# Output products of one weight block: high-part passes first, low-part passes last

## The reference, cut to what matters

```python
x = irfft(soft_threshold(rfft(x) @ (w_r, w_i) + b))   # 2 x 3008 x 256
h = x @ w_in;  g = max(h, 0) + alpha * min(h, 0);  x = g @ w_out         # layer 1, 256 -> 2048 -> 256
h = x @ w_in;  g = h if h >= 1, 0 if h <= -1, else (h + 1)**2 / 4; out = g @ w_out   # layer 2
```

## Time and profile before

| What | Value |
|---|---|
| Median of 3 runs | 1186.69 us (1186.18 to 1186.71) |
| The profiled execution: its own time | 1185.84 us |
| Its span | 1184.0 us |
| PE busy | 1172.3 us, 99% of the span |
| DVE, ACT, POOL busy | 885.6, 852.2, 693.0 us |
| Passes on TensorE | 6948 |

### The profile page before, as it was taken

The page is one execution under the profiler, slowest core; times in us unless marked ns, Lnnn a source line. Parts: engine busy times, 40 slices in busy tenths (PEclk is TensorE's granted clock), DMA queues, the critical chain, the costliest instruction groups (busy, mean ns, idle before and its releaser), DMA issues.

```text
span 1184.0 us, 21005 instructions
## 1 busy us (share of the span) xinstructions
PE 1172.3 (99%) x6948; PEld 1134.6 (96%) x6948; DVE 885.6 (75%) x1680; ACT 852.2 (72%) x1879; POOL 693.0 (59%) x724
## 2 busy tenths in 40 slices
PE   8999999999999999999999999999999999999998
PEld 2799999999999999999999999999999999999998
DVE  4687777777777777777778777777777787878775
ACT  2335567777777777777767788888878787878776
POOL 3006647667575766666556566665657575756553
PEclk9999999999999999999999999999999999999999
DMA  8687620211111201202005500000000000000000
GB/s 298 232 272 243 195 63 18 77 41 54 41 58 63 68 28 41 93 29 68 19 1 179 191 23 2 27 1 27 1 28 1 27 1 27 1 27 1 14 14 27
DMA packets 41580, 77.61 MB, mean 66 GB/s; under 512 B 4608, under 2 KB 21120, under 8 KB 41472
## 3 DMA queue, kind: packets, MB, share of 16 engines
q1 hardware_dynamic: 39392, 69.78, 17.6%
q10 hardware_dynamic: 2080, 6.48, 1.6%
HBM read 45.97 MB, written 30.28 MB: 64 GB/s over the span
## 4 chain that ended last, share of the span: by engine, by line
PE 93%; POOL 3%; DMA 1%; SPq 1%; issue 1%; ACT 1%; DVE 0%; POOLq 0%; ACTq 0%
PE bank L1170 81%; PE bank L1137 6%; PE bank L1156 2%; PE bank L1147 2%; PE bank L1122 2%; POOL g_lo L519 2%; DMA x_sb<-x 1%; POOL x_sb L465 1%; PE bank L1111 1%; POOL prep_raw L545 0%; SPq L328 0%; POOL xc_lo L495 0%; ACT prep_hi L798 0%; ACT g_hi L775 0%; SPq L334 0%
## 5 line engine op out<-in xcount | busy, mean ns | idle before, releaser
L519 POOL TENSOR_TENSOR g_lo<-g_sb,g_hi 128x376 fp32r<-128x376 f32 x510 | 506.3, 1004 | 365.8 <-ACT g_hi L775 365.2
L1170 PE MATMUL bank<-g_hi,w_out_hi 128*128 128x376 f32 x1024 | 344.9, 337 | 0.9 <-POOL g_lo L519 0.4
L1170 PE MATMUL bank<-g_lo,w_out_hi 128*128 128x376 f32 x1024 | 341.9, 334 | 0.0
L1170 PE MATMUL bank<-g_hi,w_out_lo 128*128 128x376 f32 x1024 | 341.7, 334 | 0.0
L1170 PE MATMUL bank<-xc_hi,w_in_hi 128*128 128x376 f32 x896 | 302.0, 337 | 0.0
L1170 PE MATMUL bank<-xc_hi,w_in_lo 128*128 128x376 f32 x896 | 300.3, 335 | 0.0
L1170 PE MATMUL bank<-xc_lo,w_in_hi 128*128 128x376 f32 x896 | 298.5, 333 | 0.0
L775 ACT ACTIVATE g_hi<-g_sb 128x376 fp32r<-128x376 f32 x512 | 261.1, 510 | 42.7 <-DVE g_sb L976 27.3
L1170 PEld LDWEIGHTS bank<-g_hi,w_out_hi 128*128 128x128 f32 x1024 | 192.4, 188 | 9.1 <-POOL g_lo L519 7.4
L1170 PEld LDWEIGHTS bank<-g_hi,w_out_lo 128*128 128x128 f32 x1024 | 192.4, 188 | 0.0
L1170 PEld LDWEIGHTS bank<-g_lo,w_out_hi 128*128 128x128 f32 x1024 | 192.3, 188 | 0.0
(11 more groups left out here) (83 smaller groups left out, 1534.5 us busy)
## 6 DMA issues: line engine op xcount, KB each, us to landing
gc<-group_consts SPq DMA_DIRECT2D x24, 256.0 KB, 4.4
zt<-slots_scratch SPq DMA_DIRECT2D x24, 256.0 KB, 3.8
inverse_scratch<-v_sb SPq DMA_DIRECT2D x24, 256.0 KB, 2.9
ut<-inverse_scratch SPq DMA_DIRECT2D x16, 384.0 KB, 5.1
slots_scratch<-a_sb ACTq DMA_DIRECT2D x15, 384.0 KB, 4.6
out<-y_tile SPq DMA_DIRECT2D x30, 188.0 KB, 1.9
prep_raw<-wpack SPq DMA_DIRECT2D x16, 256.0 KB, 2.6
x_sb<-x SPq DMA_DIRECT2D x15, 256.0 KB, 4.6
```

Source lines behind the costliest of these rows:

```text
L519: pool.tensor_tensor(g_lo[kind][:, :], g_sb[n % 3][:, :], g_hi[kind][:, :].bitcast(f32), ALU.subtract)\
L1170: done = pe.matmul(out_ap, w, g, start=first and n == 0, stop=last_one and n == 2, skip_group_check=unchecked)
```

## The change

`make_out` no longer works through one channel half and then the other. It goes through six pairs (c, n), c the channel half and n the pass: both high-data passes of half 0, both of half 1, then the low-data pass of half 0 and that of half 1. The first pass waits for `hi_ready`, and the wait for `lo_ready` moves ahead of the fifth pass. In the last output block of the last group the passes are sorted back into the old order, with the wait for `lo_ready` ahead of the third pass. The wait for `acc_left` of half 1 now stands ahead of the third pass and not the fourth. The helper `products` goes away; `product`, used by p1 to p7, issues the same three passes as before. The passes of the output blocks now also carry `skip_group_check`, which only concerns the building of the program.

```diff
-                pe.wait_ge(lo_ready, block_no(g, kind) + 1)
-                for c in range(DC):
-                    if first and q:
+                passes = [(0, 0), (0, 1), (1, 0), (1, 1), (0, 2), (1, 2)]
+                if (g, nth) == (ALL_GROUPS - 1, 3):
+                    passes.sort()
+                pe.wait_ge(hi_ready, block_no(g, kind) + 1)
+                for c, n in passes:
+                    if first and q and n == 0:
                         pe.wait_ge(acc_left[k][c], q)
-                    cols = slice(upper * D + c * P, upper * D + (c + 1) * P)
-                    last = products(acc_bank[k][c][:, 0:N], (w_out_hi[:, fp, cols], w_out_lo[:, fp, cols]),
-                                    (g_hi[kind][:, :], g_lo[kind][:, :]), first, last_one)
-                    if (g, nth, c) == (ALL_GROUPS - 1, 3, 0):
+                    if (c, n) == (0, 2):
+                        pe.wait_ge(lo_ready, block_no(g, kind) + 1)
+                    w, g_part = ((w_out_hi, g_hi), (w_out_lo, g_hi), (w_out_hi, g_lo))[n]
+                    last = pe.matmul(acc_bank[k][c][:, 0:N], w[:, fp, upper * D + c * P:upper * D + (c + 1) * P],
+                                     g_part[kind][:, :], start=first and n == 0, stop=last_one and n == 2,
+                                     skip_group_check=True)
+                    if (g, nth, c, n) == (ALL_GROUPS - 1, 3, 0, 2):
                         last.then_inc(last_begun, 1)
                 last.then_inc(out_done, 1)
```

More of the change, by code:

```diff
@@ L1165, in side_free @@
                 pe.wait_ge(t_made, 4 * q + (0, 0, 1, 3, 4)[jobs])
[L1167 to L1172, removed]
             def product(g, bank_of, w, xs, first=True, last_one=True):
                 q, fp = divmod(g, FP)
-                cols = slice(w * P, (w + 1) * P)
-                return products(bank_of[:, 0:N], (w_in_hi[:, fp, cols], w_in_lo[:, fp, cols]),
-                                (xc_hi[q % 2][:, xs, :], xc_lo[q % 2][:, xs, :]), first, last_one, True)
+                terms = ((w_in_hi, xc_hi), (w_in_lo, xc_hi), (w_in_hi, xc_lo))
+                for n, (w_part, x_part) in enumerate(terms):
+                    done = pe.matmul(bank_of[:, 0:N], w_part[:, fp, w * P:(w + 1) * P], x_part[q % 2][:, xs, :],
+                                     start=first and n == 0, stop=last_one and n == 2, skip_group_check=True)
+                return done
             def low_part(q, which):
```

## The result

The changed kernel takes 1182.2 us (median of 7 runs, 1181.91 to 1183.96) against 1186.69 us (7 runs) before: ratio 0.9969, 95% interval 0.9959 to 0.9979. The forecast was 1181.4 us. The profiled execution's span is 1180.1 us against 1184.0.

A forecast was written before the change was run, and what follows sets the result against it. TensorE, busy 99% of the span, was taken as the bound, losing time at stops for GpSimd's `g_lo`. Gains of 2.2 us (layer 1), 2.6 (layer 2) and 0.5 (last group), together 5.3, gave 1181.4 us; range 1176.5 to 1187.5.

The forecast's parts named there:

- The wait for the low part: Output blocks: asking for the low part four passes later gives 0.68 us of room, enough for all 43 late blocks.
- rival B: Engines working in turn bind the block; layer 2 keeps 7.806 us a group, 1184.0 to 1186.7 us; chance 0.16.
- The wait for the high part: New wait at a block's first load: high part ready 0.7 us or more ahead in ordinary blocks, cost nothing.
- 512 waits more: Additional waits carried by weight loads, no instruction added: 0 to 0.5 us, taken as 0.
- The last group: Stop at C22's block goes, later blocks stay in time, and the whole 0.48 us arrives at the end.
- The pace between the stops: Layer 2 groups run 7.760 us without stops, faster only after a stop; 7.806 before, so 2.6 us gained.
- The order of banks and factors: Output blocks' new pass order, three bank changes instead of one: between -4.9 and +4.9 us, taken as 0.
- `acc_left` of half 1: Wait one pass earlier, in 14 tile pairs twice; its copies start several us before, so cost 0.
- A: Fast pace everywhere: the new order runs all groups at 7.687 us, 1173.2 us; chance 0.12 including cases towards it.
- C: Bank alternation costs 9 ns at each of 1536 seams, 13.8 us in all, giving 1195.2 us; chance 0.14.
- D: Closer bank alternation makes TensorE's clock swing; a slow group takes 7.7 us more, ten give 1258 us; chance 0.02.
- The signs: Changed profile: `g_lo` row gone or under 0.5 us, no late block 1 pass, even 7.76 us groups, full clock.

The follow-up runs named there:

- e4_more_waits: The changed kernel with one more wait, already met, ahead of each of p1 to p7 in every group; 1182.48 us.
- e2_old_order: The changed kernel with its passes back in the old order, half by half, the low part's wait ahead of the third pass; 1180.13 us.
- e8_swapped: The e2_old_order kernel with the places of the two xc buffers (even and odd tile pairs) exchanged; 1179.52 us in one run.
- e1_order_only: The changed kernel with the wait for the low part put back ahead of all six passes; 1188.21 us.
- e11_one_change_less: The changed kernel with its two last passes exchanged, so a block changes bank twice and not three times; 1182.10 us.
- e12_five_changes: The changed kernel with the two halves taking turns at every pass, five bank changes a block in place of three; 1183.60 us.

## Why the prediction was right, and where not

**The wait for the low part.** Right. All stops at C21 are gone, in layer 1 too, and with them the row of waits; no p load behind group 0 took their place, so nothing of rival B was seen. The reading of the waits was too short, though. The seven `tokens` loads were not all that waited besides `g_lo`: the loads of the Fourier part waited over 10 us for DMA, outside the stream, and two p loads at group 0 waited 0.3 and 0.2 us for VectorE. Blocks with a late first or second pass are 41 in the trace, not 43, and the 692.89 and 693.07 us read there are not among.

**The wait for the high part, and 512 waits more.** Both 0, as shown by the missing rows and by `e4_more_waits`.

**The last group.** 0.46 us against 0.48.

**The pace between the stops.** This reading failed. I took the fast groups of layer 2 for an after-effect of a stop, from 12 of 12 that followed one, and let layer 2 gain 2.6 us. The runs showed two paces tied to the buffers of even and odd tile pairs (`e2_old_order`, `e8_swapped`), and no fast group behind a stop in `e1_order_only`; the waits alone gain 4.9 us there. The trace of before held the warning: its layer 1 has fast groups (15 and 16) that follow no stop, and in the odd pairs of layer 2 groups 73, 89, 91 and 105 follow a stop and take 7.76 us. Every fast group counted did follow a stop, but not every group behind a stop was fast.

**"The order of banks and factors: I take 0."** The term that was mis-sized. It costs 2.0 us in layer 2 (480.8 against 478.9 in `e2_old_order`; 0.3 of them are `acc_left`, below) and 0.8 in layer 1, inside the stated bounds of -4.9 to +4.9. In layer 2 the reading above had put the gain 2.3 us too low, and this cost took 2.0 us back: that the sum there came out near 2.6 is luck. In layer 1 it is half of why 0.75 us came in place of 2.2: `e2_old_order` has 1.5 there. Of the 0.7 us that are then still missing some 0.4 belong to group 0: 0.17 us of its stop lay ahead of its first output pass, and part of the rest comes back in the wait for VectorE's `g_sb`, 0.4 in place of 0.2 us. The old order with its smaller room also keeps a part of the stops in groups 5, 22, 29 and 46. That no row showed a dependence on the bank was right, `e11_one_change_less` and `e12_five_changes` confirm it; the dependence is on the moving factors' sequence and place, which I had not looked for.

**`acc_left` of half 1.** Called 0, is 0.3 us, in the eight tile pairs of layer 2. The wait stands in 15 tile pairs, not 14. "Starts several us before" was said of the copies without a row; VectorE's copy L989 ends 0.05 us before the load at group 64.

**The rivals.** A's pace of 7.687 for all did not come, but a padded new order comes near it (7.693 and 7.707, 1177.9 us). C was right in kind, an order with a price, but at a fifth of its size (2.8 of 13.8 us) and with another cause: bank changes cost nothing. D: the granted clock stayed full in all 40 slices, and in `e12_five_changes` no slower pace appeared with five bank changes in a block. The swings that the Trainium skill ("TensorE: Matmul & The Clock Gate", section "A second HAM failure mode: psum-queue depth-cycling") reports go with frequent short idling of the engine between the groups; in the changed kernel's layer 2 no weight load stands among the waits, so these runs do not test the rule. The chances of faster and slower were added up 0.01 too high and too low; the parts give 0.71 and 0.11.

**The signs.** All four that were named appeared: the row gone, no late pass at block 1, an even 7.75 us in layer 2, the clock full. The third appeared for another reason than the one given, so it could not tell the wrong reading from a right one.

## What to carry to other kernels

Where a stream on TensorE waits for a late second part, move the wait to the first instruction that reads that part, and check what else stands on the instructions that come forward with it. When TensorE never idles, compare the time of equal work between iterations: here a pace that repeated within 1 ns from group to group and changed with the buffer's parity went with where the operands lay, and not with waits. A reordering of matmuls then has to be measured together with its layout, since either order can be the better one.

## What the runs showed of the hardware

The distance between passes of the same shape (128 weights, 376 columns of 4 bytes) runs from 165 to 182 ns in the undisturbed groups of these traces, in patterns that repeat from group to group, with a mean of 170.8 to 172.6 ns that depends on the places of the moving operands in SBUF and, by elimination, on their sequence: exchanging two pairs of buffers exchanged the paces, 32 bytes of padding moved a group's time by up to 0.06 us, and neither seven more waits a group nor two, three or five bank changes a block moved it. What in SBUF or TensorE makes the pattern was not found. A weight load that started 0.10 us late (685.00 in the timeline of group 64) did not delay its own pass; the pass behind it came 0.04 us late.
